# Transposing the expert tiles' inputs on TensorE instead of VectorE

## The reference

```python
# 1: a causal convolution of 7 taps per head (8 heads), weights softmaxed
w = softmax(weight)                      # (8, 7)
out = einsum('hk,bskhg->bshg', w, x_unf)

# 2: mixture of experts, for tokens with a positive skip score
do = (x @ w_skip) > 0
logits = x[do] @ w_gate                  # 8 experts, the best one is taken
y = gate * (relu(x[do] @ w1[e]) @ w2[e]) # 192 -> 1024 -> 192
x[do] += y

# 3: a second mixture over all tokens, with another gate
x = gate * sigmoid(x @ w_output_gate)[e] * (relu(x @ w1[e]) @ w2[e])
```

## Time and profile before

| | |
|---|---|
| median of 3 runs | 1147.45 us (1146.74 to 1147.9) |
| profiled execution, its own time | 1146.74 us |
| its span, first to last instruction | 1145.0 us |
| mean granted TensorE clock | 0.977 |
| busy share: PE, DVE, ACT, POOL | 96%, 62%, 47%, 35% |

### The profile page before, as it was taken

How to read it: one execution, slowest core, us unless ns; L and a number is a source line. 1 busy time by engine, 2 the same in 40 slices (tenths; PEclk the granted TensorE clock), 3 DMA queues, 4 the chain that set the end, 5 groups by cost and what they waited for, 6 DMA issues and landing times.

```text
span 1145.0 us, 31473 instructions
## 1 busy us (share of the span) xinstructions
PE 1093.9 (96%) x8258; PEld 995.5 (87%) x8259; DVE 713.0 (62%) x2260; ACT 540.0 (47%) x1190; POOL 397.6 (35%) x435
## 2 busy tenths in 40 slices
PE   7999995799999999999969999999999999999997
PEld 5556554699999999999869999999999999999997
DVE  2445654488878888888846555565656556555554
ACT  2544552254444445445425455454545455455443
POOL 4477777223232333333313222232232223223212
PEclk9999997899999999999979999999999999999999
DMA  6854424443333443443334343443434344332232
GB/s 178 240 163 128 149 77 131 95 94 87 79 91 76 104 96 82 98 99 90 81 106 113 69 105 80 95 97 65 114 84 116 70 92 97 65 60 62 61 70 48
DMA packets 252578, 111.92 MB, mean 98 GB/s; under 512 B 168643, under 2 KB 247270, under 8 KB 252560
## 3 DMA queue, kind: packets, MB, share of 16 engines
q1 hardware_dynamic: 210784, 63.49, 26.9%
q0 software_dynamic: 15328, 27.96, 7.3%
q10 hardware_dynamic: 26448, 20.28, 6.4%
HBM read 80.49 MB, written 33.08 MB: 99 GB/s over the span
## 4 chain that ended last, share of the span: by engine, by line
PE 84%; issue 6%; POOL 5%; DVE 2%; DMA 1%; ACTq 1%; POOLq 0%; ACT 0%; SPq 0%; DVEq 0%
PE bank L1089 31%; PE bank L1104 26%; PE bank L1111 12%; PE bank L1080 5%; POOL buckets L432 5%; PE bank L1051 2%; PE bank L947 1%; PE bank L1050 1%; PE bank L1022 1%; PE bank L1023 1%; PE bank L1039 1%; PE bank L1040 1%; DMA buckets<-rows,slot_i 0%; PE bank L1013 0%; DVE kern_pad L656 0%
## 5 line engine op out<-in xcount | busy, mean ns | idle before, releaser
L1104 PE MATMUL bank<-w,hh 128*128 128x384 f32 x1488 | 444.4, 361 | 0.5 <-DVE hl L809 0.5
L1111 PE MATMUL bank<-w,hl 128*128 128x192 f32 x1488 | 363.7, 255 | 0.0
L809 DVE SCALAR_TENSOR_TENSOR hl<-bank,hh 128x512 fp32r<-128x512 f32 x372 | 252.7, 689 | 129.6 <-ACT hh L599 128.4
L599 ACT ACTIVATE hh<-bank 128x512 fp32r<-128x512 f32 x372 | 221.6, 599 | 162.6 <-PE bank L1089 156.8
L1111 PEld LDWEIGHTS bank<-w,hl 128*128 128x128 f32 x1488 | 282.8, 191 | 0.0
L1104 PEld LDWEIGHTS bank<-w,hh 128*128 128x128 f32 x1488 | 280.2, 188 | 1.6 <-DVE hl L809 0.7
L458 POOL DMA_INDIRECT out<-y_rows,out_i x120 | 117.3, 978 | 413.2 <-DVE out_i L887 381.9
L1089 PE MATMUL bank<-xAh,w1h 128*128 128x256 f32 x744 | 222.6, 299 | 0.0
L1089 PE MATMUL bank<-xAh,w1l 128*128 128x256 f32 x744 | 209.5, 282 | 0.0
L1089 PE MATMUL bank<-xB,w1h 128*128 128x256 f32 x744 | 209.2, 281 | 0.0
L1089 PE MATMUL bank<-xAl,w1h 128*128 128x256 f32 x744 | 208.9, 281 | 0.0
(11 more groups left out here) (157 smaller groups left out, 1437.5 us busy)
## 6 DMA issues: line engine op xcount, KB each, us to landing
xblocks<-buckets SPq DMA_DIRECT2D x570, 32.0 KB
xkeep<-buckets ACTq DMA_DIRECT2D x93, 196.0 KB, 2.8
raw<-w_all SPq DMA_DIRECT2D x56, 192.0 KB
xwin<-x SPq DMA_DIRECT2D x12, 768.0 KB, 5.7
raw<-w_all SPq DMA_DIRECT2D x56, 128.0 KB
raw<-w_all SPq DMA_DIRECT2D x112, 64.0 KB
xwin<-x SPq DMA_DIRECT2D x5, 672.0 KB
buckets<-rows,slot_i POOLq DMA_INDIRECT x128
```

The lines of the kernel that those rows point to most:

```text
L599: nc.scalar.activation(hh[:, 2 * c:2 * c + 2, :].rearrange("p c t -> p (c t)"), bank[c][:], ACT.Relu).then_inc(s["h_high"], 1)
L809: nc.vector.scalar_tensor_tensor(hl[:, 2 * c:2 * c + 2, :].rearrange("p c t -> p (c t)"), bank[c][:], 0.0, h, ALU.max, ALU.subtract).then_ ...
L1104: return nc.tensor.matmul(bank[Y[h]][:, 0:2 * D], hh[:, j, t], w2[:, par, j, :, :].rearrange("p a d -> p (a d)"), start=(j == 0), stop=(j ...
L1111: last = nc.tensor.matmul(bank[Y[h]][:, 0:D], hl[:, j, t], w2[:, par, j, 0, :], start=False, stop=False)
```

## The change

`x_turn` on VectorE is gone. The tile is loaded with its rows on partitions (two rows of the bucket on each), features 128 to 191 twice, by two DMAs in place of six. TensorE turns it with four transposes into bank 5 of PSUM, from where ScalarE and VectorE read it. The four stand between the h matmuls (and `scores`) and the y matmuls of the tile before. `x_trans` is now raised by TensorE, and SyncE waits for `xT_ready` (after `x_low`) in place of `x_trans`. `tile_rows`, by which `xkeep` is loaded, puts rows 2p and 2p + 1 on partition p too, in place of p and p + 128.

```diff
         def tile_rows(g, off):
-            return bass.AP(buckets.tensor, (g * T + off) * ROW, [[ROW, 128], [128 * ROW, SUB], [1, ROW]])
+            return bass.AP(buckets.tensor, (g * T + off) * ROW, [[SUB * ROW, 128], [1, SUB * ROW]])
...
                 def load_prep(g, off):
-                    for a in range(XB):
-                        p = a % 4 * 32
-                        sp.dma_start(xblocks[p:p + 32, a // 4, :].rearrange("p (b i) -> p b i", i=32),
-                                     bass.AP(buckets.tensor, (g * T + off) * ROW + a * 32,
-                                             [[ROW, 32], [32 * ROW, T // 32], [1, 32]])).then_inc(s["prep_in"], 16)
+                    for dst, src, n in ((0, 0, D), (D, 128, DB)):
+                        sp.dma_start(xprep[:, :, dst:dst + n],
+                                     bass.AP(buckets.tensor, (g * T + off) * ROW + src,
+                                             [[SUB * ROW, 128], [ROW, SUB], [1, n]])).then_inc(s["prep_in"], 16)
...
-                                sp.wait_ge(s["x_trans"], g)
+                                sp.wait_ge(s["xT_ready"], g + 1)
                                 load_prep(g, off)
...
                     act.wait_ge(s["x_trans"], n + 1)
-                    nc.scalar.copy(xAh[:], xT[:, 0, :]).then_inc(s["x_high"], 1)
-                    nc.scalar.copy(xB[0:64, :], xT[0:64, 1, :]).then_inc(s["x_high"], 1)
-                    nc.scalar.copy(xC[64:128, :], xT[0:64, 1, :]).then_inc(s["x_high"], 1)
+                    nc.scalar.copy(xAh[:], bank[5][:, 0:T]).then_inc(s["x_high"], 1)
+                    nc.scalar.copy(xC[:], bank[5][:, T:2 * T]).then_inc(s["x_high"], 1)
+                    nc.scalar.copy(xB[0:64, :], bank[5][0:64, T:2 * T]).then_inc(s["x_high"], 1)
...
-                def x_turn(n):
-
-                    dve.wait_ge(s["prep_in"], n * (16 * XB) + 16 * XB)
-                    nc.vector.transpose(xT[:, 0, :], xblocks[:, 0, :])
-                    nc.vector.transpose(xT[0:64, 1, :], xblocks[0:64, 1, :]).then_inc(s["x_trans"], 1)
-
                 def x_low(n):
 
                     dve.wait_ge(s["x_high"], n * 3 + 3)
-                    nc.vector.tensor_tensor(xAl[:], xT[:, 0, :], xAh[:].bitcast(F32), ALU.subtract)
-                    nc.vector.tensor_tensor(xB[64:128, :], xT[0:64, 1, :], xB[0:64, :].bitcast(F32),
+                    nc.vector.tensor_tensor(xAl[:], bank[5][:, 0:T], xAh[:].bitcast(F32), ALU.subtract)
+                    nc.vector.tensor_tensor(xB[64:128, :], bank[5][64:128, T:2 * T], xC[64:128, :].bitcast(F32),
                                             ALU.subtract).then_inc(s["xT_ready"], 1)
...
+                def transpose_x(n):
+
+                    pe.wait_ge(s["prep_in"], n * 32 + 32)
+                    for h in range(SUB):
+                        nc.tensor.transpose(bank[5][:, h * 128:(h + 1) * 128], xprep[:, h, 0:128], ident[:])
+                        last = nc.tensor.transpose(bank[5][:, T + h * 128:T + (h + 1) * 128],
+                                                   xprep[:, h, 128:D + DB], ident[:])
+                    last.then_inc(s["x_trans"], 1)
+
...
+                transpose_x(0)
                 pe.wait_ge(tables_ready, m + 1)
...
-                                                         w1l[k0, par, 1, at * 128:(at + 1) * 128], (xB, xC)[rows_at][k0, :],
+                                                         w1l[k0, par, 1, at * 128:(at + 1) * 128], xC[k0, :],
...
                             if m == 0:
                                 scores(g)
+                            transpose_x(g + 1)
                             pe.wait_ge(s["yrows_ready"], g + 1)
```

More of the change, by code:

```diff
@@ L56, in program @@
     MAXT = N // T + E
-    XB = D // 32
     assert S % (W * WPG) == 0 and GPB == 4 and DB == 64 and SUB == 2 and PAIRS == 4
@@ L139, in program @@
         w2 = sb("w2", [128, 2, FC, 2, D], F32R)
-        xblocks = sb("xblocks", [128, 2, T])
-        xT = sb("xT", [128, 2, T])
+        xprep = sb("xprep", [128, SUB, D + DB])
         xkeep = sb("xkeep", [128, SUB, ROW])
@@ L333, in _ @@
                     n0 = last_tile(sp, 0)
-                    sp.wait_ge(mix_sems[0]["x_trans"], n0 + 1)
+                    sp.wait_ge(mix_sems[0]["xT_ready"], n0 + 2)
                     settle(sp)
@@ L386, in _ @@
                 n = last_tile(sp, m)
-                sp.wait_ge(s["x_trans"], n)
+                sp.wait_ge(s["xT_ready"], n + 1)
                 load_prep(0, m * E * CAP)
@@ L391, in _ @@
             settle(sp)
-            sp.wait_ge(mix_sems[1]["prep_in"], n1 * (16 * XB) + 16 * XB)
+            sp.wait_ge(mix_sems[1]["prep_in"], n1 * 32 + 32)
             settle(sp)
@@ L603, in _ @@
                                     act.wait_ge(s["yrows_ready"], g + 1)
-                                    act.dma_start(xkeep[:], tile_rows(g, off)
+                                    act.dma_start(xkeep[:].rearrange("p s c -> p (s c)"), tile_rows(g, off)
                                                   ).then_inc(s["keep_in"], 16)
@@ L892, in _ @@
                     prime(dve, s["yrows_ready"])
-                x_turn(0)
                 x_low(0)
@@ L917, in _ @@
                                     pieces.one()
-                            x_turn(g + 1)
                             if m == 0:
```

## The result

The changed kernel takes 1185.64 us (median of 4 runs, 1185.27 to 1186.28) where the kernel before takes 1147.68 us beside it: 1.0339 times as long, 95% interval 1.0322 to 1.0355. That is 38.0 us more; 1187.4 was forecast. Over all its executions on record the changed kernel takes 1185.22 to 1189.61 us. Ratios and intervals are made from the fast executions of each kernel (a few of the kernel before, more than 1.5% above its fastest, are left out further on), so they are not exactly the quotient of the medians.

What follows compares the result with a forecast made beforehand. TensorE, busy throughout both loops, was taken as the bound. 1146.74 + 41.6 for transposes - 0.3 - 1.0 at the edges = 1187.0, said as 1187.4 us for the median; range of this case 1182 to 1197.

Steps and rivals of the forecast that it cites:

- TensorE is the bound and nothing idles at the place: In both loops TensorE is always busy, so four transposes before the y matmuls add to each of 93 tiles.
- 0.447 us for four: Price of four x transposes a tile, from how far y transposes push back TensorE's stream; 93 tiles give 41.6 us.
- The weight loads are hidden: Loading 128 weight columns per x transpose adds nothing to the 0.10 to 0.11 us step; exposed, 0.58 us more.
- the estimate of 1249 us: Time if each of four transposes in 93 tiles cost the skill's 0.275 us, 102 us in all; not the forecast.
- VectorE's relief, ScalarE's copies, x_low, 0 in the loops: In the loops, dropping VectorE's x_turn and reading x from PSUM on ScalarE and VectorE change the time by 0.
- The load is in time by 1.3 us at least: Next tile's x lands by 710.1 us, transposes want it at 711.45 or later: no TensorE wait in loops, 0.
- Edge 1: Start of m = 0: TensorE resumes earlier after tile 1's load but has more y matmuls left; gain 0.3 us.
- Edge 2: Start of m = 1: first matmul 1.9 us earlier, then tile 1's load is late; gain taken as 1.0 us.
- A: x transposes in the loops dearer than inserted y transposes: 1215 us at 0.74 us a tile; chance 0.10.
- B: TensorE waits for the load of x in each tile: 0.3 us each gives +28, 1215 us; chance 0.06.
- C: Faster: gains at the loops' edges, 28 us at most, exceed the transposes' cost; 1138 us; chance 0.02.
- D: Transposes in the loops nearly hidden or half price, 0.23 us for four: 1167 us; chance 0.03.

Runs made afterwards that it cites:

- the transposes kept: Changed kernel with VectorE's two transposes a tile put back, on constant data into a tile nothing reads: 1186.63 us, ratio 1.0348 to the kernel before.
- seven copies in place of three: Changed kernel with three TensorE transposes a tile instead of four, seven ScalarE copies, three VectorE subtractions: 1177.38 us, ratio 1.0256 to the kernel before.
- the earlier place: Changed kernel with the x transposes in m = 1 after half of the h matmuls instead of all: 1262.35 us, ratio 1.026 to the kernel before.
- the earlier issue: Changed kernel with SyncE waiting for x_trans, not xT_ready, before issuing the load of x: 1252.37 us, ratio 1.022 to the kernel before.

## Why the prediction was right, step by step

*TensorE is the bound and nothing idles at the place:* right. Periods grew by the transposes and nothing gave it back, and taking them out of the loop brought 9.19 us back.

*0.447 us for four:* right in m = 1 (0.446). In m = 0 it was mis-sized, 0.40. The rows of both kernels say why. Before, in m = 0 and in m = 1:

```profile
410.53 0.44 PE L1104 MATMUL bank<-w,hh 128*128 128x384 f32 x1
410.81 0.25 PE L1111 MATMUL bank<-w,hl 128*128 128x192 f32 x1
...
711.45 0.34 PE L1104 MATMUL bank<-w,hh 128*128 128x384 f32 x1
711.62 0.25 PE L1111 MATMUL bank<-w,hl 128*128 128x192 f32 x1
```

After, in m = 0:

```profile
418.06 0.33 PE L1028 MATMUL bank<-ident,xprep 128*128 128x128 f32 x1
...
418.48 0.42 PE L1104 MATMUL bank<-w,hh 128*128 128x384 f32 x1
418.73 0.25 PE L1111 MATMUL bank<-w,hl 128*128 128x192 f32 x1
```

Before, the step from the first L1104 to the next matmul took 0.28 us in m = 0, behind the matmuls of `scores`, and 0.17 in m = 1: the longer first step, which the y matmuls have behind transposes too (0.26 in m = 1 now), was already paid in m = 0. After, four transposes and the first L1104 take 0.67 us in m = 0 where that L1104 took 0.28 before, 0.39 more. This is read from the two traces, and no experiment tried it alone. It makes the sum 33 x 0.40 + 60 x 0.447 = 40.0 and not 41.6 us.

*The weight loads are hidden:* right; all four load 128 columns (142 ns), and steps stay at 0.11 us. The figure of the Trainium skill (TensorE: Matmul & The Clock Gate, Part 4: PE-mode transpose), about 275 ns and for bf16, agrees with what this trace shows as duration (0.27 us); paid in full it gave the estimate of 1249 us, which the measurement leaves out. Eight transposes and three show what is paid: 0.43 us for four more, 0.11 to 0.12 for one less.

*VectorE's relief, ScalarE's copies, x_low, 0 in the loops:* right, shown by the transposes kept, the loop without TensorE's, and seven copies in place of three.

*The load is in time by 1.3 us at least:* right, with more room. Two DMAs take 3.55 and 4.18 us from first issue to use where TensorE waits for them (205.23 to 208.78, 599.68 to 603.86), and in m = 1 there are 6.9 us (issue at 731.88, wanted at 738.77). Twice the loads fit, five times don't.

*Edge 1, a gain of 0.3 us:* a loss of 0.3. The load came at 208.78, not at 207.3 to 208.0: the second of the two DMAs goes out 0.84 us after the first and not 0.5, and takes 2.7 us; the first went out 0.5 us later too (205.23 against 204.74).

*Edge 2, a gain of 1.0 us:* 1.65, and mostly not by the path described. The new order gives 1.3 us of the 1.9 forecast: from the last `ranks` of m = 0 to the first matmul of m = 1 are 4.57 us against 5.87. Another 1.1 us stand ahead of that, where the forecast had nothing, from TensorE's last turning of y to the last `ranks`, before and after:

```profile
572.83:578.40 5.57, 3.33 (x13) 2.62 (x13) 1.66 (x11) 0.66 (x3) 1.49 (x2) 0.50 0.11 38
```

```profile
586.23:590.71 4.48, 2.02 (x13) 1.58 (x13) 1.88 (x11) 0.66 (x3) 1.49 (x2) 0.83 0.13 47
```

The granted clock there was 0.83 instead of 0.50. It is not tied to the change, as the kernel with three transposes has the same order and took 5.56 us at 0.50. The load of tile 1 was then used 4.18 us after its first issue, where 2.6 to 3.3 were reckoned, but it went out some 1.8 us earlier than reckoned, counted from the last tile of m = 0 with its transposes taken off. The sum of the edges, -1.3 forecast and -1.2 found, is right by luck: misses of both signs cancel, and the clock of one execution is among them.

*The rivals.* A, dearer transposes, is out by the traces. B, waits for the load in each tile, did not happen; it needs some 3 us more delay. Its price is then higher than I gave: with five loads the waits came with a granted clock of 0.91 in m = 1. C, edges that return more than the transposes take, would have needed 40 us where 1.2 were found. D is out: a transpose costs the step of 0.11 us, twice the 0.058 us of 128 columns at the rate of L1089.

What stays open: what slows the two other chips, by 55 to 67 us ahead of the first tile alone, and why kernels with the six small loads have longer tiles there (up to 13.49 us in m = 0 and 10.26 in m = 1) while those with two loads keep nearer to their period (at most 0.45 us over it in m = 0). That the loads are the cause was not tried. If they are, the change costs less there than the 3.1% that 38 us would be: the kernels with the earlier place and the earlier issue take 1.026 and 1.022 times the kernel before, with intervals that reach 1.034 and 1.030.

## What to carry to other kernels

When one engine is busy for the whole of a loop, expect work moved onto it to be paid in full, and relief of engines that wait for it to buy nothing; look for an idle gap at the very place before moving anything there. Take the price of an instruction from how far it pushes the stream back at a place where the same one already stands, not from its duration. A load that an engine now awaits directly is safe only as long as its issue, its landing and its queue fit in one period: compare those, and look separately at the first tiles, where nothing runs ahead.

## What was not expected

Each of the two loads holds the queue longer than one of six did: 0.70 us a DMA (1.39 for two) against 0.48 (2.90 for six), so 1.35 to 1.39 us a tile where about 1.0 was forecast. With loads five times, TensorE's waits in m = 1 reached 7.4 us, although the DMA engines were busy only 59% of the time there. (The longest wait of all, 15.2 us, is in tile 0 of m = 0, and 6.2 us of it passed before the first of the ten DMAs was issued.)

```profile
640.00:1400.00 760.00, 642.23 (x4544) 611.42 (x4543) 286.44 (x628) 264.99 (x598) 148.38 (x151) 0.91 0.59 151
```
